# First MLP of a fused attention and mixture kernel: the second product six tiles behind the first instead of four

## The chip, the cores and the metric

The kernel runs on one core of a Trainium2 chip. The metric is device microseconds of the execution; the median of three runs is compared. The engines of the core run their own instruction streams and meet at semaphores: TensorE (PE in the rows) for matrix products, VectorE (DVE), ScalarE (ACT), GpSimd (POOL), and SyncE (SP), which issues most transfers.

## What is computed

The input passes through three stages in one launch: a banded attention, a first MLP with a smooth gate, and a mixture of four experts. Cut to what matters:

```python
x = attention(q, k, v)            # 2 x 8 heads, 768 rows of 64, a band of 96 and 8 global keys
x = x.reshape(1536, 512)

h = x @ w_in                      # 512 -> 2048
g = h * tanh(softplus(h))
x = g @ w_out                     # 2048 -> 512

p = domain_probs / (domain_probs.sum(-1, keepdims=True) + 1e-9)
out = 0
for e in range(4):
    out += p[:, e:e+1] * (relu(x @ w1[e]) @ w2[e])      # 512 -> 1024 -> 512
```

All of it is float32. The kernel splits each operand into a high and a low half in float16 and sums three products (high x high, high x low, low x high).

## The kernel before

**Stages.** After the attention (the banded branch is the one that runs) the function `rest` of each engine does the MLP and the mixture. The 1536 tokens are three blocks of 512 (`NG`), called g; the hidden width of 2048 is 16 tiles of 128 (`FT`), called f. A step number T = 16 g + f counts the 48 tiles (`STEPS`). F(T) is the first product of tile T, S(T) its second product; E(f) is the first product of tile f of expert 0 for block 0.

**TensorE.** In step T it issues F(T) (`first_product`, 12 matmuls with 512 columns, result in bank T % 4), then, from step `LAG` on, S(T - LAG) (`second_product`, 12 matmuls that add to banks 4 to 7, one for each 128 of the 512 outputs). In steps 0 and 2 it also turns the attention's output for blocks 1 and 2 (`TURN_AT`). F(T) waits until VectorE has read bank T % 4 for tile T - 4 (`b_ready`), S(T) until the gated tile is ready in both halves (`h_ready`). S(0) also waits for all blocks of x to be split (`x_ready`). The first S of the next block, S(16) and S(32), also waits until ScalarE has taken the finished block out of banks 4 to 7 (`x2_taken`). Behind F(47), in steps 48 to 47 + `LAG`, E(0), E(1), ... stand in F's place (the drain of the lag); `expert_group(0, 0, LAG)` begins with the rest of them. From then on the mixture is products alone, in order of experts and blocks.

**The gate of one tile** runs over four engines. For tile T: ScalarE's exponential (L939); VectorE L1297, L1299 and L1303 (which reads the bank); ScalarE's logarithm and exponential (L953, L955); VectorE L1315 and L1317; GpSimd's product g(T) (L790); ScalarE's high half (L947); VectorE's low half (L1309). Each engine takes these in a fixed order: in its step T, VectorE does L1297, L1299 and L1303 for tile T, L1309 for tile T - 2, L1315 and L1317 for tile T - 1; so g(T) follows VectorE's step T + 1. ScalarE in its step T does L939 for tile T, L947 for tile T - 2, L953 and L955 for tile T - 1.

**Between two blocks.** `x2_due(T, after)` gives the block and a count n in steps T = `LAG` + `after` + 16 (g + 1) + n. By it, in step `LAG` + 16 (g + 1), ScalarE copies the finished block (`take_x2`, L911, four copies) ahead of that step's own exponential; VectorE takes the maximum of each quarter in four steps from there (`x2_max`, L1248), SyncE sends it to memory and back to all partitions, VectorE makes the scale seven steps later (`x2_scale`) and ScalarE and VectorE make the halves of the block for the experts (`x2_high` L902, `x2_low` L1240) from eight steps later. Other work in these steps has numbers of its own that don't depend on `LAG`: the pieces of the maximum of expert 0's weights (L1028, steps 6 to 20), the scales of expert 0 (step 25), and its halves (L920 and L1273, steps 32 to 42 and 48 to 51).

The lines on which the turn from one block to the next hangs are these. In `second_product` (TensorE) and in ScalarE's loop:

```python
                    for d in range(DC):
                        if f == 0 and g > 0:
                            pe.wait_ge(x2_taken, DC * (g - 1) + d + 1)
...
                for T in range(STEPS + LAG):
                    taken = x2_due(T, 0)
                    if taken and taken[1] == 0:
                        take_x2(taken[0])
                    if T < STEPS:
                        act.wait_ge(h_psum, T + 1)
```

The ring of gated tiles, `hv`, has 8 places (`RING`); ScalarE's high half of tile m waits for S(m - 8) (`l2_done`).

Of the kernel before, what the change touches and what calls it, by code (L numbers as in the profile page):

```python
# [36 lines left out]
def program(nc, q, k, v, n_global, n_local, w_in, w_out, probs, w1, w2, out):  # L37
# [6 lines left out]
    DC = DM // P  # L44
    FT = FF // P
    ET = FE // P
    GT = 4
    GN = GT * P
    NG = N // GN
# [23 lines left out]
    with ExitStack() as ctx:  # L73
# [30 lines left out]
        def psum(i, n=GN, at=0):  # L104

            c = 512 * (i % 2) + at
            return bank[i // 2][:, c:c + n]
# [183 lines left out]
        accv = acc[:].rearrange("p (t f) -> p t f", t=NT)  # L291

        STEPS = NG * FT
        LAG = 4


        TURN_AT = {0: 1, 2: 2}
# [31 lines left out]
        def x2_due(T, after):  # L329

            g, n = divmod(T - LAG - after, FT)
            return (g - 1, n) if 1 <= g <= NG else None
# [147 lines left out]
        def _(pe):  # L480
# [19 lines left out]
            def turn_x(g, c):  # L500

                for j in range(GT):
                    b, t = divmod(g * GT + j, QT)
                    at = (b * DC + c) * QT * P + t * P
                    last = pe.transpose(psum(x_bank(g, c), P, j * P), acc[:, at:at + P], ident[:])
                last.then_inc(xT_psum, 1)
# [118 lines left out]
            def rest():  # L625
# [21 lines left out]
                def second_product(T):  # L647

                    g, f = divmod(T, FT)
                    if T == 0:  # L650
                        pe.wait_ge(x_ready, XN)
                        pe.wait_ge(w_split, 2)
                    pe.wait_ge(h_ready, T + 1)
# [3 lines that stand above are left out]
                        for n, (a, b) in enumerate(((0, 0), (0, 1), (1, 0))):  # L657
                            last = pe.matmul(psum(4 + d), w_out_s[:, a, f // 2, f % 2, d * P:(d + 1) * P], hv[:, T % RING, b, :],  # L658
                                             start=(f == 0 and n == 0), stop=(f == FT - 1 and n == 2))
                        if f == FT - 1:  # L660
                            last.then_inc(x2_psum, 1)
                    if f < FT - 1:
                        last.then_inc(l2_done, 1)
                    else:
                        pe.sem_inc(l2_done, 1)
# [15 lines left out]
                def expert_group(e, g, begun=0):  # L681

                    _, w2_s = expert(e)
                    for f in range(begun, ET):
                        expert_first(e, g, f)
                    if isinstance(g, int):
                        pe.wait_ge(x2_taken, DC * NG)
                        pe.wait_ge(w0_lo, PIECES)
                    for j in range(GT):

                        pe.wait_ge(y_added, NT * e + GT * g + j + 1)
                        split_product(psum(4 + j), lambda c, s: hv[:, c, s, j * P:(j + 1) * P],
                                      lambda c, s: w2_s[:, s, c, :], ET,
                                      (lambda c: pe.wait_ge(f_ready, ET * (NG * e + g) + c + 1)) if j == 0 else None,
                                      ).then_inc(y_psum, 1)

                pe.wait_ge(x_ready, DC)
                pe.wait_ge(w_split, 1)
                for T in range(STEPS + LAG):
                    if T < STEPS:  # L700
# [3 lines left out]
                    if T in TURN_AT:  # L704
                        pe.wait_ge(x_ready, DC * TURN_AT[T])
                        for c in range(DC):
                            turn_x(TURN_AT[T], c)
                    if T >= LAG:
                        second_product(T - LAG)

                expert_group(0, 0, LAG)
                with pe.Fori(1, NG) as g:
# [93 lines left out]
        def _(act):  # L806
# [89 lines left out]
            def rest():  # L896
# [33 lines left out]

                for T in range(STEPS + LAG):
                    taken = x2_due(T, 0)
# [49 lines left out]
        def _(dve):  # L982
            def chain(done, before=0):


                n = [0]

                def link(ins):
                    n[0] += 1
                    ins.then_inc(done, 1)  # L990
                    dve.wait_ge(done, before + n[0])

                return link
# [29 lines left out]
            def weights_part(n, c):  # L1023

                if c in (0, PIECES // 2):
                    dve.wait_ge(w2_loaded if c else w1_loaded, 16 * (n - 1))
                at = c * PIECE
                dve.tensor_reduce(wpieces[:, c:c + 1], stage[:, at:at + PIECE], AX_X, ALU.max,  # L1028
                                  apply_absolute_value=True).then_inc(w_piece, 1)
# [195 lines left out]
            def rest():  # L1225
# [11 lines left out]
                def x2_low(g, c):  # L1237

                    dve.wait_ge(x_hi, XN + DC * g + c + 1)
                    dve.scalar_tensor_tensor(xs(g, c, 1), y32[:, c], scale_cols(SC_X2)[2], xs(g, c, 0),  # L1240
                                             ALU.mult, ALU.subtract).then_inc(x_ready, 1)
# [3 lines left out]
                def x2_max(g, c):  # L1245

                    dve.wait_ge(x2_taken, DC * g + c + 1)
                    last = dve.tensor_reduce(part[:, c:c + 1], y32[:, c], AX_X, ALU.max, apply_absolute_value=True)  # L1248
                    if c == DC - 1:
                        chain(x2_step, X2_STEPS * g)(last)  # L1250
                        dve.tensor_reduce(part[:, 4:5], part[:, 0:4], AX_X, ALU.max).then_inc(xmax_ready, 1)
# [24 lines left out]
                def expert_scales(e):  # L1276
                    link = chain(scale_step, 4 * SCALE_STEPS + 2 + (2 * SCALE_STEPS + 3) * e)
                    dve.wait_ge(max_in, 16 * (1 + e))
                    for j, s in ((0, SC_W1), (1, SC_W2)):
                        link(dve.tensor_reduce(scale_cols(s + e % 2)[0],  # L1280
                                               rows[1][:].rearrange("p (q m) -> p m q", m=2)[:, j], AX_X, ALU.max))
                        make_scale(link, scale_cols(s + e % 2))
                    dve.sem_inc(w_scale, 1)  # L1283
                    link(dve.tensor_tensor(inv_e[:, e % 2:e % 2 + 1], scale_cols(SC_W1 + e % 2)[3],
                                           scale_cols(SC_W2 + e % 2)[3], ALU.mult))

                def expert_low(e, g, f):

                    dve.wait_ge(f_hi, ET * (NG * e + g) + f + 1)
                    dve.scalar_tensor_tensor(hv[:, f, 1, :], psum(f % 4), 0.0, hv[:, f, 0, :],  # L1290
                                             ALU.max, ALU.subtract).then_inc(f_ready, 1)
# [49 lines left out]
                def expert_group(e, g, begun=0):  # L1341

                    share = pr[:].rearrange("p (t e) -> p e t", e=E)[:, e, g * GT:(g + 1) * GT]
                    dve.wait_ge(y_added, GT + NT * e + GT * g)
                    dve.tensor_scalar(pg[:], share, inv_g[:, g:g + 1], inv_e[:, e % 2:e % 2 + 1],
                                      ALU.mult, ALU.mult).then_inc(pg_ready, 1)
                    for f in range(begun, ET):
                        expert_low(e, g, f)
                        if (e, g) == (0, 0):
                            x2_max(NG - 1, f - begun)  # L1350
                        if (e, g) == (0, 1) and f >= ET - DC:
                            x2_low(NG - 1, f - ET + DC)
                    if g == 1 and e + 1 < E:
                        expert_scales(e + 1)
                    dve.wait_ge(pg_ready, NG * e + g + 1)
                    for j in range(GT):
                        if g == 0 and e + 1 < E:

                            for c in range(PIECES // GT):
                                weights_part(3 + e, PIECES // GT * j + c)  # L1360
                        dve.wait_ge(y_psum, NT * e + GT * g + j + 1)
                        y = acc[:, (g * GT + j) * DM:(g * GT + j + 1) * DM]
                        if e == 0:
                            last = dve.tensor_scalar(y, psum(4 + j), pg[:, j:j + 1], None, ALU.mult)
                        else:
                            last = dve.scalar_tensor_tensor(y, psum(4 + j), pg[:, j:j + 1], y, ALU.mult, ALU.add)  # L1366
                        last.then_inc(y_added, 1)
                    if g == 0 and e + 1 < E:
                        weights_max(3 + e)
                    if (e, g) == (0, 0):  # L1370
                        x2_scale(NG - 1)
# [48 lines left out]
```

## Time and profile before

| | us |
|---|---|
| median of 3 runs | 915.09 |
| lowest, highest | 912.17, 916.41 |
| the profiled execution | 915.88 |
| its span in the profile | 913.8 |

The profiled execution's own time is 2.1 us more than its span, which counts from the first instruction to the last. In the span the attention ends near 154 us, the first MLP's products run from there to about 423 us, and the mixture takes the rest. The page of the profile gives the busy time of each engine; a timeline gives each run of like instructions with its start, its duration and, in brackets, the idle time before it with the instruction that ended it. A matmul's recorded end lies a little past the next one's start, so that the length of a product is best read from the start of one row to the start of the next.

### The profile page before, as it was taken

The page shows a single profiled execution, that of the slowest core. Times are in us where ns is not written, and L with a number is a line of the kernel's source. Part 1 is how long each engine was busy: PE and PEld are TensorE (multiplying, and loading weights), DVE is VectorE, ACT ScalarE, POOL GpSimd, SP SyncE. Part 2 cuts the span into 40 slices and gives each one's busy share as a digit, 9 for nine tenths or more (in the row PEclk, how much of TensorE's full clock was granted, in tenths as well). Part 3 has the DMA queues.
Part 4 walks back from the last instruction along what each step waited for, and adds up shares of the span by engine and source line. Part 5 has one row for each costly group of instructions (what it writes and reads, how often), then busy time and mean ns, then how long its engine had stood idle before and what let it go on. Part 6 is the DMA issues. An engine that isn't in the chain of part 4 may idle for free.

```text
span 913.8 us, 12568 instructions
## 1 busy us (share of the span) xinstructions
PE 873.1 (96%) x4884; PEld 441.3 (48%) x4884; DVE 506.8 (55%) x1016; ACT 315.7 (35%) x591; POOL 266.0 (29%) x218
## 2 busy tenths in 40 slices
PE   3878998999999999999999999999999999999998
PEld 3766786444444444444444444444444444444443
DVE  7855876999999999996642225322134322212121
ACT  3699885545454555454030111101020101101020
POOL 1266994122222232320009500059000193000000
PEclk8798999999999999999999999999999999999999
DMA  9762340000000000202000400000400000000001
GB/s 220 242 220 55 82 156 1 1 1 1 0 1 10 1 0 1 78 18 93 4 6 0 151 34 0 7 1 2 182 1 0 6 0 0 1 24 23 34 12 49
DMA packets 52005, 39.20 MB, mean 43 GB/s; under 512 B 40816, under 2 KB 41712, under 8 KB 51440
## 3 DMA queue, kind: packets, MB, share of 16 engines
q1 hardware_dynamic: 49888, 34.31, 12.5%
q10 hardware_dynamic: 2064, 4.19, 1.3%
q8 instruction: 31, 0.51, 0.3%
q14 instruction: 22, 0.18, 0.1%
HBM read 35.35 MB, written 3.15 MB: 42 GB/s over the span
## 4 chain that ended last, share of the span: by engine, by line
PE 69%; DVE 21%; ACT 7%; issue 2%; DMA 0%; POOL 0%; DVEq 0%; SPq 0%; ACTq 0%
PE bank L635 58%; PE bank L658 5%; DVE tmp L1299 4%; DVE tmp L1317 3%; PE bank L540 2%; DVE xT L1315 2%; DVE tmp L1297 2%; PE bank L566 2%; DVE tmp L1303 2%; ACT scaled L841 2%; PE bank L585 1%; DVE hid L1309 1%; ACT tmp L824 1%; ACT tmp L858 1%; ACT tmp L953 1%
## 5 line engine op out<-in xcount | busy, mean ns | idle before, releaser
L927 ACT ACTIVATE hid<-bank 128x512 f16<-128x512 f32 x96 | 57.3, 596 | 410.6 <-PE bank L635 410.6
L635 PE MATMUL bank<-xT,wA 128*128 128x512 f16 (+1 forms) x864 | 196.2, 381 | 1.1 <-DVE acc L1114 1.1
L1290 DVE SCALAR_TENSOR_TENSOR hid<-bank,hid 128x512 f16<-128x512 f32 x96 | 66.4, 692 | 172.3 <-ACT hid L927 172.3
L658 PE MATMUL bank<-hid,wB 128*128 128x512 f16 x576 | 132.2, 379 | 4.4 <-ACT acc L911 2.6
L635 PEld LDWEIGHTS bank<-xT,wA 128*128 128x128 f16 x864 | 84.8, 98 | 103.7 <-issue 2.2
L790 POOL TENSOR_TENSOR tmp<-tmp 128x512 f32<-128x512 f32 x48 | 70.1, 1460 | 198.2 <-DVE tmp L1317 198.2
L635 PE MATMUL bank<-wA,hid 128*128 128x512 f16 x576 | 125.3, 379 | 0.0
L635 PE MATMUL bank<-xT,wB 128*128 x576 | 125.3, 379 | 0.0
L635 PE MATMUL bank<-wB,hid 128*128 128x512 f16 x576 | 125.3, 379 | 0.0
L745 POOL TENSOR_SCALAR stage<-stage,sc 128x1024 f32<-128x1024 f32 x32 | 35.9, 1120 | 252.8 <-DVEq L1283 240.8
L1366 DVE SCALAR_TENSOR_TENSOR acc<-bank,pg,acc 128x512 f32<-128x512 f32 x36 | 27.0, 751 | 131.7 <-PE bank L635 131.7
L658 PEld LDWEIGHTS bank<-hid,wB 128*128 128x128 f16 x576 | 56.1, 98 | 73.0 <-DVE hid L1309 3.6
L635 PEld LDWEIGHTS bank<-wA,hid 128*128 128x128 f16 x576 | 56.4, 98 | 67.9
L635 PEld LDWEIGHTS bank<-xT,wB 128*128 128x128 f16 x576 | 56.4, 98 | 68.0
L635 PEld LDWEIGHTS bank<-wB,hid 128*128 128x128 f16 x576 | 56.4, 98 | 68.0
L947 ACT ACTIVATE hid<-tmp 128x512 f16<-128x512 f32 x48 | 30.2, 630 | 107.8 <-POOL tmp L790 106.0
L1184 DVE SCALAR_TENSOR_TENSOR tmp<-bank,tmp 128x384 f16<-128x384 f32 (+2 forms) x96 | 47.0, 490 | 30.5 <-ACT tmp L858 29.4
L635 PE MATMUL bank<-xT,hid 128*128 (+1 forms) x288 | 63.3, 379 | 0.0
L824 ACT ACTIVATE tmp<-tmp 128x288 f32<-128x288 f32 (+2 forms) x96 | 48.7, 507 | 20.3 <-DVE tmp L1074 18.8
L566 PE MATMUL bank<-ident,tmp 128*128 128x128 f32 x240 | 47.4, 299 | 6.0 <-DVE tmp L1184 3.3
L1299 DVE SCALAR_TENSOR_TENSOR tmp<-tmp 128x512 f32<-128x512 f32 x48 | 48.4, 1007 | 1.6
L540 PE MATMUL bank<-hid 64*128 64x256 f32 (+2 forms) x320 | 39.7, 360 | 9.1 <-DVE tmp L1074 8.2
(110 smaller groups left out, 930.6 us busy)
## 6 DMA issues: line engine op xcount, KB each, us to landing
stage<-in_moe_w SPq DMA_DIRECT2D x8, 2048.0 KB, 9.1
stage<-in_moe_w_in SPq DMA_DIRECT2D x1, 4096.0 KB, 14.2
wB<-in_moe_w_out ACTq DMA_DIRECT2D x1, 4096.0 KB, 15.9
hid<-in_q SPq DMA_DIRECT2D x16, 192.0 KB, 3.2
hid<-in_k SPq DMA_DIRECT2D x16, 192.0 KB, 3.4
xT<-in_v SPq DMA_DIRECT2D x8, 384.0 KB, 5.1
out_y<-acc SPq DMA_DIRECT2D x12, 256.0 KB, 2.0
rows<-max SPq DMA_DIRECT2D x4, 128.0 KB, 4.2
```

What stands on the lines that cost most here:

```text
L540: last = pe.matmul(*parts[a][n], start=True, stop=True)
L566: last = pe.transpose(dst[:, b * P:(b + 1) * P], src[:, b * P:(b + 1) * P], ident[:])
L635: last = pe.matmul(dst, lhs(c, a), rhs(c, b), start=(c == 0 and n == 0), stop=(c == chunks - 1 and n == 2))
L658: last = pe.matmul(psum(4 + d), w_out_s[:, a, f // 2, f % 2, d * P:(d + 1) * P], hv[:, T % RING, b, :], start=(f == 0 and n == 0), stop=(f ...
L745: pool.tensor_scalar(tmp, src, scale, 1.0, ALU.mult, ALU.mult).then_inc(w_part, 1)
L790: pool.tensor_tensor(g_t[T % 4], g_t[T % 4], r_t[T % 2], ALU.mult).then_inc(g_ready, 1)
L824: act.activation(t, t, ACT.Exp, bias=nmax[:, u:u + 1], scale=-1.0).then_inc(p_ready, 1)
L927: act.activation(hv[:, f, 0, :], psum(f % 4), ACT.Relu).then_inc(f_hi, 1)
L947: act.activation(hv[:, m % RING, 0, :], g_t[m % 4], ACT.Copy).then_inc(h_hi, 1)
L1184: dve.scalar_tensor_tensor(pt[:, 1], src, P_SCALE, pt[:, 0], ALU.mult, ALU.subtract).then_inc(pT_dve, 1)
L1290: dve.scalar_tensor_tensor(hv[:, f, 1, :], psum(f % 4), 0.0, hv[:, f, 0, :], ALU.max, ALU.subtract).then_inc(f_ready, 1)
L1299: dve.scalar_tensor_tensor(n, u, 2.0, u, ALU.add, ALU.mult).then_inc(n_ready, 1)
```

## The change

`LAG` becomes 6. F(4) and F(5) are then issued with no second product behind them, F(6) comes ahead of S(0), and six tiles of expert 0 instead of four stand in the drain. Whatever is tied to `LAG` moves by two steps on each engine: the copies of a finished block, its maxima, its scale and its halves, and the shares of the mixture (step 8 instead of 6). The maxima of the last block stand among the remaining tiles of expert 0; with two tiles left instead of four, one maximum stands behind E(6) and three behind E(7).

```diff
         STEPS = NG * FT
-        LAG = 4
+        LAG = 6
...
                     for f in range(begun, ET):
                         expert_low(e, g, f)
                         if (e, g) == (0, 0):
-                            x2_max(NG - 1, f - begun)
+                            for c in range(DC):
+                                if f == min(begun + c, ET - 1):
+                                    x2_max(NG - 1, c)
```

How the instructions stand on TensorE at the start of the MLP before the change (x12 is one product, L635 a first product, L658 a second one, L505 a block of x being turned):

```order
L505 MATMUL bank<-ident,acc 128x128 x16
L635 MATMUL bank<-xT,wA 128x512 x24
L658 MATMUL bank<-hid,wB 128x512 x12
L635 MATMUL bank<-xT,wA 128x512 x12
L658 MATMUL bank<-hid,wB 128x512 x12
```

and after it:

```order
L505 MATMUL bank<-ident,acc 128x128 x16
L635 MATMUL bank<-xT,wA 128x512 x48
L658 MATMUL bank<-hid,wB 128x512 x12
L635 MATMUL bank<-xT,wA 128x512 x12
L658 MATMUL bank<-hid,wB 128x512 x12
```

Two first products more stand ahead of the first second product: F(3) to F(6) instead of F(3) and F(4).

On ScalarE at the end of block 0, the difference between the two orders (L911 are the copies of the finished block, the four others the work of one step):

```order
 L953 ACTIVATE tmp<-tmp,sc 128x512
 L955 ACTIVATE tmp<-tmp 128x512
+L939 ACTIVATE tmp<-bank,sc 128x512
+L947 ACTIVATE hid<-tmp 128x512
+L953 ACTIVATE tmp<-tmp,sc 128x512
+L955 ACTIVATE tmp<-tmp 128x512
+L939 ACTIVATE tmp<-bank,sc 128x512
+L947 ACTIVATE hid<-tmp 128x512
+L953 ACTIVATE tmp<-tmp,sc 128x512
+L955 ACTIVATE tmp<-tmp 128x512
 L911 COPY acc<-bank 128x512 x4
 L939 ACTIVATE tmp<-bank,sc 128x512
```

The copies stand behind steps 20 and 21, ahead of the exponential of step 22; they stood ahead of that of step 20.

On VectorE in step 33 (L1240 is a low half of block 0's output, L1273 one of expert 0's weights):

```order
 L1317 SCALAR_TENSOR_TENSOR tmp<-xT,tmp 128x512
 L1240 SCALAR_TENSOR_TENSOR xT<-acc,sc,xT 128x512
+L1273 SCALAR_TENSOR_TENSOR hid<-stage,sc,hid 128x1024
 L1297 TENSOR_SCALAR tmp<-tmp 128x512
 L1299 SCALAR_TENSOR_TENSOR tmp<-tmp 128x512
```

The two kinds, which had steps of their own, meet in this step, since only the first moves with `LAG`.

## Rows read from the trace of the kernel before

**Rows 1.** Page, part 1: busy us and share of the span of each engine.

```profile
PE 873.1 (96%) x4884; PEld 441.3 (48%) x4884; DVE 506.8 (55%) x1016; ACT 315.7 (35%) x591; POOL 266.0 (29%) x218
```

**Rows 2.** Timeline, TensorE, first MLP: start us, us, line, operation, [idle before, releaser].

```profile
154.04 4.43 PE L635 MATMUL bank<-xT,wA 128*128 128x512 f16 x12 [1.08 <-DVE acc L1114]
158.31 1.91 PE L505 MATMUL bank<-ident,acc 128*128 128x128 f32 x16
...
166.99 5.34 PE L635 MATMUL bank<-xT,wA 128*128 128x512 f16 x24
174.08 2.76 PE L658 MATMUL bank<-hid,wB 128*128 128x512 f16 x12 [1.75 <-DVE xT L1169]
176.68 2.75 PE L635 MATMUL bank<-xT,wA 128*128 128x512 f16 x12
...
207.76 2.75 PE L635 MATMUL bank<-xT,wA 128*128 128x512 f16 x12
```

**Rows 3.** Timeline, TensorE, S(16) and S(32).

```profile
257.60 2.75 PE L658 MATMUL bank<-hid,wB 128*128 128x512 f16 x12 [0.47 <-ACT acc L911]
...
342.79 2.75 PE L658 MATMUL bank<-hid,wB 128*128 128x512 f16 x12 [2.15 <-ACT acc L911]
```

**Rows 4.** Chain that ended last, in order of time: its last long piece.

```profile
423.24 486.93 PE bank L635 x2256
```

**Rows 5.** Timeline, VectorE: a plain step, and tile 7's L1303.

```profile
182.50 0.42 DVE L1297 TENSOR_SCALAR tmp<-tmp 128x512 f32<-128x512 f32 x1
182.95 1.64 DVE L1299 SCALAR_TENSOR_TENSOR tmp<-tmp 128x512 f32<-128x512 f32 x1
...
187.35 0.42 DVE L1297 TENSOR_SCALAR tmp<-tmp 128x512 f32<-128x512 f32 x1
...
196.57 0.69 DVE L1303 SCALAR_TENSOR_TENSOR tmp<-bank,tmp 128x512 f32<-128x512 f32 x1
```

**Rows 6.** Timeline, VectorE, steps 32 and 33: the low halves.

```profile
327.12 0.74 DVE L1240 SCALAR_TENSOR_TENSOR xT<-acc,sc,xT 128x512 f16<-128x512 f32 x1
...
332.64 1.28 DVE L1273 SCALAR_TENSOR_TENSOR hid<-stage,sc,hid 128x1024 f16<-128x1024 f32 x1
333.83 1.50 DVE L1297 TENSOR_SCALAR tmp<-tmp 128x512 f32<-128x512 f32 x1
```

**Rows 7.** Timeline, GpSimd: g(17) to g(21), g(33), g(35).

```profile
253.77 1.27 POOL L790 TENSOR_TENSOR tmp<-tmp 128x512 f32<-128x512 f32 x1 [3.46 <-DVE tmp L1317]
258.86 1.27 POOL L790 TENSOR_TENSOR tmp<-tmp 128x512 f32<-128x512 f32 x1 [3.81 <-DVE tmp L1317]
263.93 1.27 POOL L790 TENSOR_TENSOR tmp<-tmp 128x512 f32<-128x512 f32 x1 [3.81 <-DVE tmp L1317]
269.44 1.27 POOL L790 TENSOR_TENSOR tmp<-tmp 128x512 f32<-128x512 f32 x1 [4.24 <-DVE tmp L1317]
274.51 1.26 POOL L790 TENSOR_TENSOR tmp<-tmp 128x512 f32<-128x512 f32 x1 [3.81 <-DVE tmp L1317]
...
338.86 1.38 POOL L790 TENSOR_TENSOR tmp<-tmp 128x512 f32<-128x512 f32 x1 [3.81 <-DVE tmp L1317]
...
350.01 1.27 POOL L790 TENSOR_TENSOR tmp<-tmp 128x512 f32<-128x512 f32 x1 [3.81 <-DVE tmp L1317]
```

**Rows 8.** Timeline, ScalarE, around the copies of block 0.

```profile
256.89 2.03 ACT L911 COPY acc<-bank 128x512 f32<-128x512 f32 x4
258.79 0.72 ACT L939 ACTIVATE tmp<-bank,sc 128x512 f32<-128x512 f32 x1
...
262.98 0.69 ACT L939 ACTIVATE tmp<-bank,sc 128x512 f32<-128x512 f32 x1 [0.92 <-PE bank L635]
```

**Rows 9.** Timeline, VectorE, the start of step 20.

```profile
259.54 0.86 DVE L1297 TENSOR_SCALAR tmp<-tmp 128x512 f32<-128x512 f32 x1 [0.76 <-ACT tmp L939]
```

**Rows 10.** Busy by stretch: from:to us, length, busy of PE to POOL, PEclk, DMA.

```profile
150.00:154.00 4.00, 2.10 (x41) 1.66 (x38) 2.90 (x9) 1.36 (x3) 0.00 (x0) 1.00 0.02 4
154.04:157.45 3.41, 3.41 (x9) 1.18 (x10) 0.17 (x2) 0.00 (x0) 0.00 (x0) 0.50 0.00 0
```

## The prediction

> **What bounds the kernel now.** I read the busy shares first, then TensorE's timeline through the first MLP with the waits at its lines' ends, then those of the other engines where it waits, and the chain. TensorE is busy 96% of the span and VectorE 55% [rows 1], but in the first MLP VectorE is busy all the time too: its steps follow each other without a gap [rows 5]. TensorE has three waits of weight there: 1.75 us before S(0), behind VectorE's split of x [rows 2], and 0.47 and 2.15 us before S(16) and S(32), behind ScalarE's copies of the finished block [rows 3]. I call the last two the turnovers. From S(32) on TensorE never waits: after S(47) comes one unbroken piece of 486.93 us [rows 4]. So the time is set by when S(32) starts and by how much TensorE work lies behind it. Between the three no row has a wait: the gated tile itself, which the lag is there to wait for, is never late.
>
> **The pace of the two engines.** TensorE needs 2.59 us for a product of twelve matmuls (174.08 to 176.68, and 2.59 from row to row), so 5.18 us for a step [rows 2]. VectorE's plain step is 4.85 us (182.50 to 187.35) [rows 5]; 0.95 us of it is a hold-up while GpSimd works: L1299 takes 1.64 us where the same form takes 0.69. Extra work comes on top: a low half of x takes 0.74 us, one of expert 0 moves the next instruction by 1.19 us, and that L1297 is still held up, at 1.50 us for 0.42 [rows 6]. So VectorE gains at most 0.33 us per step on TensorE.
>
> **Part 1, the start.** Before, S(0) waits until 174.08 us. Now F(5) and F(6) go ahead of it: F(4) starts at 166.99 + 2.59 = 169.58 us, S(0) at 169.58 + 3 x 2.59 = 177.35 us, over 3 us after the split of x, which let S(0) go before. S(0) is 3.27 us later with 5.18 us more work done: a gain of 1.91 us, the wait of 1.75 us in it. The result banks don't stop F: it now runs 7.1 us earlier than before against VectorE, and the nearest case, F(11) at 207.76 us, which waits for VectorE's L1303 of tile 7, done at 196.57 + 0.69 = 197.26 us, had 10.5 us to spare [rows 2, 5].
>
> **Part 2, the first turnover.** S(16) may start only after ScalarE has copied the finished block out of the banks that S(16) writes. That copy stood at the head of ScalarE's step 20 and now stands at the head of step 22, while S(16) moves from TensorE's step 20 to its step 22: the distance between the two is as before. In ScalarE's queue the copies stand behind the high half, logarithm and exponential of the step before, and those wait for GpSimd's product g(17), which follows VectorE's step 18. In the trace g(17) starts at 253.77 us and S(16) 3.83 us later, at 257.60 [rows 3, 7]. Now it is g(19). Before, g(19) started at 263.93 us [rows 7]; VectorE had waited 0.76 us for the exponential behind the copies (256.89 to 258.79) [rows 8, 9], of which 0.22 us stayed (258.86 to 263.93 is 5.07 us for a plain 4.85, since GpSimd's product runs under the wait), and this moves on to step 22. So g(19) starts at 263.7 us and S(16) at 267.53 us. TensorE is there at 177.35 + 16 x 5.18 = 260.23 us and waits 7.3 us instead of 0.47. S(16) is 9.93 us later, with two first products (5.18 us) more done: the gain of 1.91 us has become a loss of 4.75 us. Queued behind the wait on TensorE is F(23). At full clock it ends at 267.53 + 5.18 = 272.71 us, 0.4 us earlier than before (F(21) at 257.60 + 5.18 = 262.78, and two steps of 5.18), so VectorE is as well fed as before.
>
> **Part 3, the second turnover.** Likewise S(32) follows g(33), at 338.86 us, by 3.93 us [rows 3, 7], and now has to follow g(35), at 350.01 us before. What moves on VectorE up to there is nearly even. The four maxima go from steps 20 to 23 into steps 22 to 25; so do the block's scale (29 for 27) and the low halves (31 to 34 for 29 to 32). The step in which a maximum lay beside a piece of the weights' maximum was 5.51 us long (g(19) to g(20)), the one with a maximum alone, as good as, 5.07 (g(20) to g(21)) [rows 7]: 0.44 us come back; against it the maximum that now meets the expert's scales costs its full time, by the like low half some 0.7 us, for 0.2; the low half that now shares step 33 with a low half of expert 0 costs its 0.7 us as before. That evens out within 0.1 us, and I take g(35) at 349.95 us, and S(32) at 353.88. TensorE could be there at 267.53 + 82.88 = 350.41 us, so VectorE decides again, with a wait of 3.5 us. Put shortly: VectorE's two steps up to g(35) hold 11.1 us (338.86 to 350.01, with a low half in them), TensorE's two products 5.18. Against before S(32) is 353.88 - 342.79 = 11.09 us later, and 5.18 us of first products no longer lie behind it: **+5.91 us**.
>
> **Part 4, the end.** After S(32) nothing stops TensorE. The gated tiles were never late and now have two steps more; E(4) and E(5) of expert 0 go into the lag's drain and wait for VectorE's low halves of E(0) and E(1), which lie four steps earlier. S(47) would end near 434 us instead of 423. E(6) and E(7) follow (5.18 us), and under them lie the last four copies (2.03 us, as at the first turnover [rows 8]) and the four maxima, of which three now stand in one place after E(7): under 2 us, ahead of a drain that has 2 us of room per block, cost nothing. If that cover were gone they would cost those 2 us. The load of expert 1, the shares and the DMAs of the maxima shift by at most two steps, with room of more than one step each: nothing.
>
> **Part 5, the clock.** The granted clock is at its full level (2.4 GHz) throughout the MLP but for one stretch of 3.41 us at 154.04 us, where it is 0.50 (1.2 GHz); in the 4.0 us before it TensorE had been busy for 2.10 [rows 10]. The twelve matmuls there took 4.27 us (to 158.31) [rows 2], 1.68 us more. Waits of 1.75 and 2.15 us did not bring it down. A wait of 7.3 us is idler than what did, so I take one such stretch after it. Then F(23) ends at 274.39 us, its exponential starts 0.20 us later (262.98 for the product that ended at 257.60 + 2 x 2.59 = 262.78 [rows 3, 8]), VectorE's step 0.75 us after that (258.79 to 259.54 [rows 8, 9]), at 275.34. On VectorE's own pace g(21), at 274.51 us before, comes 0.65 us earlier (0.22 and 0.44 from parts 2 and 3), and L1297 is done when GpSimd's product is, with some 0.3 us more: 273.86 + 1.26 + 0.3 = 275.42 [rows 7]; now it is at 275.76. That is 0.34 us, and the two steps after it follow TensorE's 5.18 us instead of 5.08 with little more: 0.6 us in all. The other 1.1 us lies in the 3.5 us wait of the second turnover, which falls to 2.4 us. **Sum: 5.9 + 0.6 = +6.5 us**, 915.88 to 922.4 for the profiled execution. The median of the runs lies 0.79 us lower, so 915.09 + 6.5 = 921.6 us.
>
> The Trainium skill, page "TensorE: Matmul & The Clock Gate", section "What's actually happening", says that the throttled state is the default, that activity lifts it and idleness brings it back. The rows agree as far as they go (0.50 after the thin end of the attention); without that rule the sum would be +5.9, with it +6.5. The page "SBUF — State Buffer", section "Who interferes with whom", says that VectorE with two SBUF inputs and a reading GpSimd shut each other out, and that a reduction does not. By it the moved maxima may hide under GpSimd's product and the moved low halves may not; were the low halves to hide too, the sum would be 4.8.
>
> **The rivals.**
> *All three waits go* (faster). If S(16) could follow TensorE's own arrival, 1.75 + 0.47 + 2.15 = 4.4 us are gained: 910.7 us. The mechanism is VectorE running ahead, and the place g(19): it decides from g(19) at 260.23 - 3.83 = 256.40 us, 7.3 us before what I expect. For it speaks that 0.95 us of each plain step is a hold-up by GpSimd; against it, that nothing in the change touches that, and VectorE has 0.76 us of waits to lose there. Chance 0.04.
> *The moved work is covered* (within 0.5%). The low half that meets another in step 33 falls under GpSimd's product, up to 1.07 us, the clock costs nothing and the ends of the steps fall well: 5.9 - 1.1 - 0.3 = +4.5 us, 919.6 us. For it: the maxima are partly covered now. Against it: the 1.50 us hold-up behind a low half [rows 6]. Chance 0.15.
> *The low clock lasts* (slower). Two such stretches double 1.68 us; F(23) is then 3.4 us late, VectorE 2.2 us: 5.9 + 2.2 = +8.1, 923.2 us. If the second wait brings the clock down too, up to 1.7 us more come on top. Chance 0.20 for both.
>
> **How the numbers follow.** My forecast, +6.5 us, has 0.61. The bounds are the clock (0 to 2.2, once 1.7 more) and the moved work (-1.1 to +0.5); with the median's own scatter (912.17 to 916.41) the range is 917.2 to 925.8 us, and leaves out the gain and the worst of the clock. A measurement can tell about 0.5%, 4.6 us. Slower by more: 0.78 (forecast and low clock, less some scatter); within: 0.18; faster: 0.04.
>
> **What would show it.** Before S(0) no wait, S(0) near 177.4 us; before S(16) a wait of 7 us behind L911, S(16) near 267.5; a stretch of clock 0.50 just behind it; before S(32) a wait of 2 to 4 us, S(32) near 354.5; VectorE's steps unchanged at 4.85; the last unbroken piece starting near 434.8 us. I am wrong if S(16) starts before 262 us, which would mean that the copies are not tied to VectorE's step, or if a wait shows behind S(32).

## The result and the profile after

| | before | after |
|---|---|---|
| median of 7 runs, us | 915.11 | 922.97 |
| lowest, highest, us | 912.17, 916.58 | 920.37, 924.83 |
| the profiled execution, us | 915.88 | 924.05 |
| its span, us | 913.8 | 921.9 |

The ratio of after to before is 1.0081 (95% interval 1.0064 to 1.0098): the changed kernel is 7.4 us slower (5.9 to 9.0; the two medians lie 7.9 us apart). The span of the profiled execution grew by 8.1 us.

The page's part 1 shows nothing of it at a glance: TensorE is busy for 3.0 us more, VectorE for 3.5 less [rows 1].

```profile
PE 876.1 (95%) x4884; PEld 442.1 (48%) x4884; DVE 503.3 (55%) x1016; ACT 316.9 (34%) x591; POOL 263.4 (29%) x218
```

TensorE's timeline (start us, us, what, idle before it) at the places of [rows 2, 3]:

```profile
154.17 4.45 PE L635 MATMUL bank<-xT,wA 128*128 128x512 f16 x12 [1.08 <-DVE acc L1114]
158.46 1.91 PE L505 MATMUL bank<-ident,acc 128*128 128x128 f32 x16
...
167.13 10.52 PE L635 MATMUL bank<-xT,wA 128*128 128x512 f16 x48
177.49 2.75 PE L658 MATMUL bank<-hid,wB 128*128 128x512 f16 x12
...
267.66 4.05 PE L658 MATMUL bank<-hid,wB 128*128 128x512 f16 x12 [7.12 <-ACT acc L911]
271.55 2.75 PE L635 MATMUL bank<-xT,wA 128*128 128x512 f16 x12
...
354.72 4.39 PE L658 MATMUL bank<-hid,wB 128*128 128x512 f16 x12 [2.72 <-ACT acc L911]
358.91 2.84 PE L635 MATMUL bank<-xT,wA 128*128 128x512 f16 x12
361.58 2.75 PE L658 MATMUL bank<-hid,wB 128*128 128x512 f16 x12
```

S(0) starts at 177.49 us without a wait. S(16) waits 7.12 us and S(32) 2.72 us, both behind ScalarE's copies. All of TensorE's waits in the MLP, from the view of waits, of after and then of before:

```profile
PE bank L658 <- ACT acc L911: 9.8, 2, 7.1
PE bank L635 <- DVE acc L1114: 1.1, 1, 1.1
```

```profile
PE bank L658 <- ACT acc L911: 2.6, 2, 2.2
PE bank L658 <- DVE xT L1169: 1.7, 1, 1.7
PE bank L635 <- DVE acc L1114: 1.1, 1, 1.1
```

The columns are the total in us, how often, and the longest. One wait of 1.7 us is gone and 7.2 us have come to the other two. GpSimd's rows for g(19), g(21) and g(35), to be read against [rows 7], with those of ScalarE's copies of block 0 behind them:

```profile
263.84 1.26 POOL L790 TENSOR_TENSOR tmp<-tmp 128x512 f32<-128x512 f32 x1 [3.47 <-DVE tmp L1317]
...
273.99 1.27 POOL L790 TENSOR_TENSOR tmp<-tmp 128x512 f32<-128x512 f32 x1 [3.81 <-DVE tmp L1317]
...
350.79 1.38 POOL L790 TENSOR_TENSOR tmp<-tmp 128x512 f32<-128x512 f32 x1 [3.81 <-DVE tmp L1317]
```

```profile
265.13 0.63 ACT L947 ACTIVATE hid<-tmp 128x512 f16<-128x512 f32 x1 [2.25 <-POOL tmp L790]
265.67 0.71 ACT L953 ACTIVATE tmp<-tmp,sc 128x512 f32<-128x512 f32 x1
266.41 0.63 ACT L955 ACTIVATE tmp<-tmp 128x512 f32<-128x512 f32 x1
266.95 2.03 ACT L911 COPY acc<-bank 128x512 f32<-128x512 f32 x4
```

This is the chain that holds S(16): the product g(19), then ScalarE's high half, logarithm and exponential of its step 21, then the copies; S(16) goes 3.82 us after g(19). S(32) goes 3.93 us after g(35). Then the stretches around the two waits (from:to, length, busy of PE, PEld, DVE, ACT, POOL, granted clock, DMA):

```profile
263.56:270.38 6.82, 2.72 (x7) 1.02 (x8) 5.96 (x10) 4.57 (x9) 2.53 (x2) 0.50 0.02 1
355.72:359.13 3.41, 3.41 (x10) 1.22 (x8) 2.33 (x4) 2.78 (x5) 1.18 (x1) 0.51 0.00 0
```

The granted clock is 0.50 (1.2 GHz) for 6.8 us from within the first wait on, and for another 3.4 us from 1.0 us after the start of S(32) on. S(16) takes 3.89 us instead of 2.59 (to 271.55), S(32) 4.19 (to 358.91) and the next product 2.67. The last piece of the chain, against [rows 4], is shorter by the two tiles of expert 0 that went into the drain (5.18 us) and starts 13.6 us later:

```profile
436.86 481.75 PE bank L635 x2232
```

### The profile page after: what moved, and what is told of

It reads as the page before. It is cut to its first block, busy times and chain, and to the rows that moved or that the text cites. A ratio compares the mean times of both kernels' runs of the same rounds, so it can differ in the third digit from the quotient of the medians.

```text
span 921.9 us, 12567 instructions
## 1 busy us (share of the span) xinstructions
PE 876.1 (95%) x4884; PEld 442.1 (48%) x4884; DVE 503.3 (55%) x1016; ACT 316.9 (34%) x591; POOL 263.4 (29%) x218
## 3 DMA queue, kind: packets, MB, share of 16 engines
q10 hardware_dynamic: 2064, 4.19, 1.2%
## 4 chain that ended last, share of the span: by engine, by line
PE 74%; DVE 17%; ACT 6%; issue 2%; DMA 0%; POOL 0%; DVEq 0%; SPq 0%; ACTq 0%
PE bank L635 59%; PE bank L658 7%; DVE tmp L1299 3%; PE bank L540 2%; DVE tmp L1317 2%; PE bank L566 2%; DVE xT L1315 2%; DVE tmp L1297 2%; ACT scaled L841 2%; DVE tmp L1303 2%; PE bank L585 1%; DVE hid L1309 1%; ACT tmp L824 1%; ACT tmp L858 1%; PE bank L497 1%
## 5 line engine op out<-in xcount | busy, mean ns | idle before, releaser
L635 PE MATMUL bank<-xT,wA 128*128 128x512 f16 (+1 forms) x864 | 195.9, 381 | 1.1 <-DVE acc L1114 1.1
L658 PE MATMUL bank<-hid,wB 128*128 128x512 f16 x576 | 135.1, 385 | 9.8 <-ACT acc L911 9.8
L635 PEld LDWEIGHTS bank<-xT,wA 128*128 128x128 f16 x864 | 85.0, 98 | 104.1 <-issue 3.1
L635 PE MATMUL bank<-wB,hid 128*128 128x512 f16 x576 | 125.3, 379 | 0.0
L635 PE MATMUL bank<-xT,wB 128*128 x576 | 125.3, 379 | 0.0
L635 PE MATMUL bank<-wA,hid 128*128 128x512 f16 x576 | 125.3, 379 | 0.0
L790 POOL TENSOR_TENSOR tmp<-tmp 128x512 f32<-128x512 f32 x48 | 67.5, 1407 | 201.2 <-DVE tmp L1317 201.2
L658 PEld LDWEIGHTS bank<-hid,wB 128*128 128x128 f16 x576 | 56.8, 99 | 80.2 <-DVE hid L1309 10.8
L635 PEld LDWEIGHTS bank<-wB,hid 128*128 128x128 f16 x576 | 56.4, 98 | 67.9
L635 PEld LDWEIGHTS bank<-wA,hid 128*128 128x128 f16 x576 | 56.4, 98 | 68.0
L635 PEld LDWEIGHTS bank<-xT,wB 128*128 128x128 f16 x576 | 56.3, 98 | 68.0
L635 PE MATMUL bank<-xT,hid 128*128 (+1 forms) x288 | 63.6, 379 | 0.0
```

The source lines that it names most:

```text
L635: last = pe.matmul(dst, lhs(c, a), rhs(c, b), start=(c == 0 and n == 0), stop=(c == chunks - 1 and n == 2))
L790: pool.tensor_tensor(g_t[T % 4], g_t[T % 4], r_t[T % 2], ALU.mult).then_inc(g_ready, 1)
```

## The experiments

Two theories stood against each other. **A**: the turnovers are tied, through ScalarE's queue, to VectorE's steps, so the copies' place in that queue decides; the low clock comes on top. **B**: the deeper lag costs by itself (the drain, the moved maxima and halves, the ring of gated tiles, that is, the eight places in which they stand until S has read them).

Each kernel's ratio is to runs of the kernel before that were taken along with it, so the ratios compare and the medians only roughly do. To compare executions whose attention ended at different times I give, beside them, the length of the MLP in the one profiled execution of each kernel: from the first L505 row (the end of F(0)) to the first row of expert 0's second products (wA,hid). It is 433.44 - 158.31 = 275.13 us before and 441.87 - 158.46 = 283.41 us after.

| kernel | copies in steps | MLP, us | MLP minus that of before, us | ratio to before (95%) |
|---|---|---|---|---|
| lag 4 (before) | 20, 36 | 275.13 | | |
| lag 4, copies one earlier | 19, 35 | 273.89 | -1.2 | 0.9985 (0.9973 to 0.9997) |
| lag 5 | 21, 37 | 278.74 | +3.6 | 1.0035 (1.0019 to 1.0051) |
| lag 5, copies one earlier | 20, 36 | 271.34 | -3.8 | 0.9959 (0.9946 to 0.9973) |
| lag 6 (after) | 22, 38 | 283.41 | +8.3 | 1.0081 (1.0064 to 1.0098) |
| lag 6, again | 22, 38 | 283.13 | +8.0 | 1.0087 (1.0068 to 1.0107) |
| lag 6, copies one earlier | 21, 37 | 275.74 | +0.6 | 1.0002 (0.9988 to 1.0017) |
| lag 6, copies two earlier | 20, 36 | 270.26 | -4.9 | 0.9941 (0.9921 to 0.9962) |
| lag 6, waits filled | 22, 38 | 281.03 | +5.9 | 1.0072 (1.0054 to 1.0091) |
| lag 6, expert 0's halves in 39 to 46 | 22, 38 | 281.37 | +6.2 | 1.0065 (1.0052 to 1.0078) |
| lag 6, the same in 36 to 43 | 22, 38 | 280.47 | +5.3 | 1.0061 (1.0040 to 1.0081) |

**The changed kernel once more**, as a measure on the same chip.

> The changed kernel once more, as the measure for the others on the same chip. Theory (the turnovers are tied to VectorE, the clock comes on top): 920 to 925 us, +5.9 us of waits and +0.6 to +3 us of low clock against the kernel before; S(16) near 267.6 us, S(32) near 354.6. Rival (the loss is in the drain or the mixture): the last piece of products would start within 6 us of before and the rest be lost behind it.

922.84 us. S(16) waited 7.10 us and S(32) 2.71, as in the first profile, but here the clock was at 0.50 for 10.2 us, from within the first wait to behind S(16), and stayed up after the second:

```profile
266.72 5.28 PE L658 MATMUL bank<-hid,wB 128*128 128x512 f16 x12 [7.10 <-ACT acc L911]
271.79 3.01 PE L635 MATMUL bank<-xT,wA 128*128 128x512 f16 x12
...
355.21 2.75 PE L658 MATMUL bank<-hid,wB 128*128 128x512 f16 x12 [2.71 <-ACT acc L911]
```

The waits repeat to 0.02 us; where the clock adds its part does not. Here S(16) and the next product take 2.7 us more than at full clock (266.72 to 274.63 for twice 2.59), against 1.3 us in the first profile, and S(32) takes none more. The rest of the mixture is not longer (480.0 us behind the MLP in both), against B's drain.

**The copies back in their old steps**, with the lag of six:

```diff
-                    taken = x2_due(T, 0)
-                    if taken and taken[1] == 0:
+                    taken = x2_due(T, -2)
+                    if taken and taken[1] == 0 and taken[0] < NG - 1:
```

> The changed kernel with ScalarE's copies of blocks 0 and 1 put two steps earlier in its queue, into step 20 and 36, where they stood before the change; nothing else differs. Theory (the loss is the two steps of VectorE that the copies moved behind): S(16) starts on TensorE's own arrival, 260.2 to 260.5 us, without a wait; VectorE loses about 1 us, since the exponential of step 20 waits behind the copies, which wait for S(15); S(32) at 343.1 to 343.9 us; no stretch of low clock. Sum 343.6 - 342.8 - 5.2 = -4.4 us against the kernel before, 910 to 911.5 us, 11 to 13 us under the changed kernel. Rival (the deeper lag itself costs, by the drain, the moved maxima and halves, or the ring of gated tiles): it stays above the kernel before, 917 to 922 us.

The added condition leaves the last block's copies, which stand behind the loop, where they are. 909.83 us, by the ratio 5.4 us under the kernel before and just under the expected range: the two steps of ScalarE by which the copies were moved make the difference between the slowest and the fastest kernel of the table. TensorE's only wait from the end of the attention to the end of the MLP is the 1.07 us before F(0); around S(16) its rows are:

```profile
254.33 2.75 PE L635 MATMUL bank<-xT,wA 128*128 128x512 f16 x12
256.92 2.75 PE L658 MATMUL bank<-hid,wB 128*128 128x512 f16 x12
259.51 2.75 PE L635 MATMUL bank<-xT,wA 128*128 128x512 f16 x12
```

and ScalarE's, where the copies now stand ahead of step 20's exponential:

```profile
253.57 2.03 ACT L911 COPY acc<-bank 128x512 f32<-128x512 f32 x4
255.47 0.72 ACT L939 ACTIVATE tmp<-bank,sc 128x512 f32<-128x512 f32 x1
```

VectorE waits 0.77 us for that exponential, as it did before [rows 9]. The MLP is 4.9 us shorter: the three waits of before, 4.4 us, and 0.16 us with each of them, by which the product behind a wait is later than its row shows (S(0): 1.91 us for 1.75). B would have kept the loss; everything of the deeper lag is still in this kernel.

**Lags of five**, as the change has them and with the copies in steps 20 and 36:

```diff
-        LAG = 6
+        LAG = 5
```

> A lag of five tiles instead of six, with five in the drain. Theory (each step of lag moves the copies one VectorE step on and TensorE only one first product): S(0) at 174.8 us without a wait; S(16) behind g(18), near 262.8 us, after a wait of 5.2 us; S(32) behind g(34), 347.9 to 348.8 us; 348.4 - 342.8 - 2.6 = +3.0 us against the kernel before, and 0 to 3 us of low clock: 918 to 921 us. Rival (the loss comes only with a lag beyond five, as the gain at the start is complete with five): 913 to 915 us.

> A lag of five, with the copies one step earlier in ScalarE's queue, so in steps 20 and 36 as in the kernel before. Theory: S(0) at 174.8 us without a wait, S(16) at 257.7, S(32) at 342.8 us behind a wait of 2 us, as before, but with one first product more done: -2.6 us, 912.5 us. Between the lag of four (0) and the lag of six with the copies in the same steps (-4.4 us). Rival (only the wait before S(0) is gained): -1.8 us at most and no order between the three.

918.42 and 912.19 us. The waits with the plain lag of five:

```profile
260.96 4.40 PE L658 MATMUL bank<-hid,wB 128*128 128x512 f16 x12 [4.08 <-ACT acc L911]
...
348.08 2.75 PE L658 MATMUL bank<-hid,wB 128*128 128x512 f16 x12 [2.39 <-ACT acc L911]
```

The first is 1.1 us shorter than I had said. g(18) comes earlier there, since the shares of the mixture, which go with the lag, fall into VectorE's step 7, which has no piece of the weights' maximum: from product to product on GpSimd that step takes 5.79 us (196.52 to 202.31), while with a lag of six, beside such a piece in step 8, it takes 6.91 (first fence the lag of five, second the changed kernel):

```profile
196.52 1.26 POOL L790 TENSOR_TENSOR tmp<-tmp 128x512 f32<-128x512 f32 x1 [3.81 <-DVE tmp L1317]
202.31 1.27 POOL L790 TENSOR_TENSOR tmp<-tmp 128x512 f32<-128x512 f32 x1 [4.52 <-DVE tmp L1317]
```

```profile
202.43 1.27 POOL L790 TENSOR_TENSOR tmp<-tmp 128x512 f32<-128x512 f32 x1 [3.47 <-DVE tmp L1317]
209.34 1.38 POOL L790 TENSOR_TENSOR tmp<-tmp 128x512 f32<-128x512 f32 x1 [5.65 <-DVE tmp L1317]
```

Steps 7 and 8 together, from g(6) to g(8), take 10.86 us with the lag of five and 11.76 in the changed kernel, which is 0.9 of the 1.1 us. A piece by itself (1.21 us on VectorE) makes a step only 0.23 us longer (5.08 for 4.85), one behind the shares 1.12 us (6.91 for 5.79).

With the copies one step earlier the lag of five is 3.7 us under the kernel before by the ratio (its wait before S(32) was 0.92 us, where I had expected 2), between the lags of four and six with the copies in the same steps. That a fifth tile of lag gains there is clear of the scatter; that a sixth gains more is not, since the intervals of the two ratios overlap, and only the profiles have it (1.1 us in the MLP).

**The lag of six, copies one step earlier; and the lag of four, copies one step earlier** (`x2_due(T, -1)` in both, with the same guard as above).

> The changed kernel with the copies one step earlier, in steps 21 and 37. Theory: S(16) near 262.9 us after a wait of 2.6 us, S(32) near 348.8 us after a wait of 3 us; 348.8 - 342.8 - 5.2 = +0.8 us, with 0 to 1.7 us of low clock: 915.5 to 917.5 us. So half the way between the copies in step 20 (-4.4 us) and in step 22 (+7.9 us). Rival (any lag deeper than four costs by itself): closer to the changed kernel, over 919 us.

> The kernel before (lag of four) with ScalarE's copies of blocks 0 and 1 one step earlier in its queue, in steps 19 and 35. Theory (the turnovers are tied to ScalarE's queue and through it to VectorE, whatever the lag): S(0) keeps its wait of 1.75 us; S(16) starts at 257.0 us and S(32) near 340.1 without the waits of 0.47 and 2.15 us; VectorE loses up to 2.4 us behind the exponential of step 19. Sum -2.0 to -2.7 us, 912.4 to 913.1 us. Rival (VectorE's loss comes back as a wait at the second turnover or for a gated tile): within 1 us of the kernel before.

914.91 us and 913.57 us. The first is no change (+0.2 us by the ratio, +0.6 in the MLP), 0.6 us under the range that A gave and far from B's 919. Its waits are 2.37 and 1.10 us, where 2.6 and 3 had been expected; the clock fell behind the first of them:

```profile
263.01 4.44 PE L658 MATMUL bank<-hid,wB 128*128 128x512 f16 x12 [2.37 <-ACT acc L911]
...
348.84 2.75 PE L658 MATMUL bank<-hid,wB 128*128 128x512 f16 x12 [1.10 <-ACT acc L911]
```

The second missed my expectation: a gain of 1.4 us by the ratio instead of 2.0 to 2.7. Both turnovers are free of waits there, but VectorE waits 0.98 us for the exponential behind the copies in step 19, and three gated tiles now come late (0.8 us of waits), in a kernel that had never waited for one. Two of the three:

```profile
376.77 2.76 PE L658 MATMUL bank<-hid,wB 128*128 128x512 f16 x12 [0.29 <-DVE hid L1309]
...
387.67 2.76 PE L658 MATMUL bank<-hid,wB 128*128 128x512 f16 x12 [0.36 <-DVE hid L1309]
```

So with the copies early a lag of four is too short: the rival of this run came in part, and it says what the deeper lag is good for.

**The waits filled.** Products that nobody reads keep TensorE busy in the changed kernel's waits:

```diff
+                    if f == 0 and g > 0:
+                        n = T + LAG + 1
+                        pe.wait_ge(b_ready, n - 3)
+                        for _ in range(28 if g == 1 else 12):
+                            pe.matmul(psum(n % 4), w_in_s[:, 0, 0, 0:P], xs(g, 0, 0), start=True, stop=True)
                     for d in range(DC):
```

> The changed kernel with idle products added where it waits: 28 matmuls of 512 columns ahead of S(16), 12 ahead of S(32), written to the bank that the next first product overwrites; the result is unchanged. They take 6.0 and 2.6 us of the waits. Theory (part of the loss is the low clock after the waits, 1.3 us after the first and 1.6 after the second): both stretches of clock 0.50 go, F(23) ends 1.3 us earlier, S(32) starts 0.3 to 0.9 us earlier and its product takes 2.59 us instead of 4.19: 2 to 2.5 us less than the changed kernel, +5.9 us against the kernel before. Rival (the clock costs nothing, since the second wait covers the first stretch and VectorE decides everything): within 0.5 us of the changed kernel.

921.68 us. The filling lasts 6.2 us in the first wait, under a granted clock of 1.00, and S(16) behind it has its full pace:

```profile
259.24:265.50 6.26, 6.20 (x29) 2.64 (x27) 5.96 (x9) 3.93 (x7) 1.27 (x1) 1.00 0.00 0
266.41:272.00 5.59, 5.59 (x26) 2.56 (x27) 4.73 (x8) 4.07 (x8) 1.26 (x1) 1.00 0.05 1
```

The MLP is 5.9 us over before, which is the sum without the clock. In the profiles that is 2.1 to 2.4 us less than the changed kernel, as expected; between the ratios it is 1.4 us, and their intervals overlap. So the clock's part is shown in the traces, and in the times of the runs it is not told apart from their scatter.

**VectorE relieved on the way to the second turnover.** Expert 0's low halves, which stood in steps 33 and 35, go behind g(35):

```diff
-        W0_HIGH = [32, 34, 39, 41] + [STEPS + c for c in range(PIECES // 2)]
+        W0_HIGH = [39, 41, 43, 45] + [STEPS + c for c in range(PIECES // 2)]
```

> The changed kernel with the first four halves of expert 0's weights later: ScalarE's in steps 39, 41, 43, 45 for 32, 34, 39, 41, VectorE's each one step behind. That takes two pieces of 1.19 us out of VectorE's way to the second turnover and leaves the turnovers where they are. Theory (VectorE's steps set the turnover): S(16) as in the changed kernel, near 267 us after a wait of 7.1 us; g(35) and S(32) 2.4 us earlier, near 352.4 us, the wait falls from 2.7 us to under 0.6, and no low clock follows: 2.4 to 4 us less than the changed kernel, 919 to 920.5 us. Rival (TensorE or ScalarE sets it): S(32) stays near 354.8 us and the time at 922.8.

> As the run before, but with the halves of expert 0's weights in steps 36, 38, 40, 42 (ScalarE) and 37, 39, 41, 43 (VectorE): still behind the second turnover's g(35), but early enough that E(0) does not wait for them, as it did there for 1.46 us. Theory: S(32) 2.0 us earlier than in the changed kernel, with a wait under 0.6 us, no wait before E(0), no low clock behind the second wait: 2.0 to 3.5 us less than the changed kernel, 919.5 to 921 us. Rival (what is gained at the second turnover is lost again elsewhere, as in the run before): 922 to 923 us.

922.31 us, which misses the expected 919 to 920.5, and, with [36, 38, 40, 42], 920.56 us. VectorE's halves (`W0_LOW`) stand one step behind ScalarE's, so both engines' move. The second wait falls from 2.72 us to 0.36 and 0.24:

```profile
353.14 2.75 PE L658 MATMUL bank<-hid,wB 128*128 128x512 f16 x12 [0.36 <-ACT acc L911]
403.97 2.76 PE L635 MATMUL bank<-xT,hid 128*128 128x512 f16 x12 [1.46 <-DVE hid L1273]
```

These rows are of the first of the two: the wait at S(32) is nearly gone, and a new one stands before E(0), for halves that came too late. Without it the second of the two kernels is 2.4 us under the changed one by the ratios (1.0061 against 1.0087, with intervals that overlap). Its MLP is 2.7 us shorter than that of the repeated run, whose clock was low in the same place and for as long, with the first wait at 7.10 us in both.

That it is VectorE and not ScalarE whose halves counted is seen in the changed kernel: in steps 33 to 36 VectorE's rows follow each other without a wait, while ScalarE waits for GpSimd's product in each step, which follows VectorE's L1317:

```profile
340.95 0.63 ACT L947 ACTIVATE hid<-tmp 128x512 f16<-128x512 f32 x1 [3.15 <-POOL tmp L790]
```

And the two steps from product to product that held the halves, 6.66 and 6.06 us, take 5.52 and 4.84 without them. VectorE sets the second turnover.

## Why the prediction was right

*The start* (part 1). S(0) was put at 177.35 us and came at 177.49, with everything 0.13 to 0.15 us later from F(0) on.

*The first turnover* (part 2). g(19) at 263.7 and S(16) at 267.53 were forecast; 263.84 and 267.66 came, which is exact with the shift. The wait of 7.3 us was 7.12. The place of the copies made it, as the run with the copies in step 20 shows.

*The second turnover* (part 3). By the sum 86.35 us lie between S(16) and S(32) at full clock (353.88 - 267.53); with the waits filled it was 86.46 us. In the changed kernel the low clock held F(23) back, and g(35) came at 350.79 us against 349.95 + 0.6 + 0.13 = 350.68 by the sum; S(32) followed it by 3.93 us, the very distance of before. So up to S(32) the loss was 354.72 - 342.79 - 5.18 = 6.75 us, 6.6 without the shift, against 6.5 forecast.

*The clock* (part 5) was the weak step. The first stretch was there; S(16) took 1.30 us more than at full clock where I had put 1.68, and S(32) came the forecast 0.6 us later for it (87.06 us behind S(16) for 86.46). But I had taken a second wait of 2.4 us to leave the clock up, since 2.15 us had. The second wait was 2.72 us, and behind it the clock fell: 1.68 us (1.60 in S(32) and 0.08 in the next product), all of it on the path, since no wait is left that could take it up. That is the whole difference between 6.75 and the 8.43 us (441.87 - 433.44) that the MLP became longer; the mixture gave 0.3 back to the span. It had been named as an extra on a rival of 0.20. The repeated run shows it is not in every execution: after 2.71 us the clock stayed up. But there the first stretch was the longer one, 10.2 us, and S(32) came 88.49 us behind S(16), 2.0 us later than at full clock, close to the 2.2 us of the rival in which the low clock lasts. So in both profiles the clock cost 2.0 to 2.3 us and not 0.6, each time by one half of that rival (chance 0.20), and this term of the sum was too small; the total stayed in reach because the waits, 5.9 us, are most of it. The profiled execution's 8.2 us (924.05 - 915.88) is nearer to this rival's 8.1 than to the forecast's 6.5, and the 7.4 us of the runs lies between them. With a lag of six and copies one step earlier it fell after 2.37 us, with a lag of five it stayed up after 2.39. What decides for waits of 2.4 and 2.7 us is open.

*The end* (part 4). TensorE waited for nothing behind S(32), and the three maxima after E(7) cost nothing. The last unbroken piece started at 436.86 us instead of 434.8, by the second stretch of low clock.

*The rivals.* That all three waits go would have given 910.7 us; the kernel that does it, by the place of the copies, measures 909.83. What was missing from the change was that the turnover be uncoupled from the lag. The covered work (+4.5 us) did not come about. The low half that moved into step 33 cost 0.60 us: from g(32) to g(33) it is 6.66 us (first two rows), and before, without it, 6.06:

```profile
332.55 1.71 POOL L790 TENSOR_TENSOR tmp<-tmp 128x512 f32<-128x512 f32 x1 [3.81 <-DVE tmp L1317]
339.21 1.71 POOL L790 TENSOR_TENSOR tmp<-tmp 128x512 f32<-128x512 f32 x1 [4.96 <-DVE tmp L1317]
```

```profile
332.80 2.25 POOL L790 TENSOR_TENSOR tmp<-tmp 128x512 f32<-128x512 f32 x1 [3.81 <-DVE tmp L1317]
338.86 1.38 POOL L790 TENSOR_TENSOR tmp<-tmp 128x512 f32<-128x512 f32 x1 [3.81 <-DVE tmp L1317]
```

The Trainium skill's rule on the clock (page "TensorE: Matmul & The Clock Gate", section "What's actually happening"), that idleness brings the throttled state back and activity lifts it, agrees with the filled waits: clock 1.00 with them, 0.50 without.

## What to carry to other kernels

Before you deepen a software pipeline, look up which wait each stall is: here the waits at the block ends were for an accumulator to be copied out, by an instruction that stood in the same step of another engine's queue, and the deeper lag moved that instruction behind two more steps of VectorE (10.2 us, g(17) to g(19)) while it gave TensorE only two more first products (5.2 us) to do. A lag buys slack only for waits on the lagged product itself; a copy that ends a block is better placed by when its data are complete than by the lag's step count. After the change ask again which wait is next: with the copies early, a lag of four ran into late tiles, and the lag of six then paid, 5.4 us under the kernel before.

## What the runs showed of the hardware

In the first MLP of the profiled executions the granted clock fell to 0.50 (1.2 GHz) within the waits of 7.10 to 7.12 us (four profiles with a lag of six) and within 1.0 us after waits of 4.08, 2.72 and 2.37 us, but not after 2.71, 2.39, 2.15 and 1.75. It stayed low for 3.4 to 10.2 us; in the longest case S(16), the product behind the wait, took 5.07 us (266.72 to 271.79) for 2.59, nearly wholly at half pace. With products added in the waits it stayed at 1.00.

A later wait took up only part of what the low clock cost TensorE, in both profiles 0.7 us: of 1.3 us the start of S(32) kept 0.6, of 2.7 us 2.0, and the wait there was 2.7 us each time, since VectorE had become late as well (in the repeated run g(21) to g(22) took 6.47 us, for 5.07 with the waits filled). Behind the last wait all 1.68 us counted.

What an operation adds to a VectorE step that GpSimd's product holds up depends on what it is: a reduction of 1.21 us behind L1317 added 0.23 us (5.08 for 4.85 us), a low half of 0.74 us added 0.67 (5.52).
